# Order of a load queue: keys of the second tile against pieces of weights

## The reference, cut to what matters

```python
out_d = sm_attn(q_d, k_d, v_d)            # q, k, v averaged over 4 positions
out_up = np.repeat(out_d, factor, axis=2)
mask = np.abs(pos[:, None] - pos[None, :]) < factor
...
out_local = np.matmul(attn, v)
x = out_up + out_local                    # to (2304, 512)
xn = x / rms * rms_g
x = (silu(xn @ w_gate) * (xn @ w_val)) @ w_out          # 512 -> 1536 -> 512
r = np.maximum(x @ w_in, 0.0)
out = (s * (r * r) + b) @ w_out2                        # 512 -> 2048 -> 512
```

## Time and profile before

| | |
|---|---|
| runs | 1056.06, 1056.22, 1058.25 us; median 1056.22 |
| the profiled execution | 1057.01 us, of which 1054.9 us are the span of the trace |
| PE busy | 968.6 us (92%) |
| DVE, ACT, POOL busy | 529.8, 329.9 and 411.5 us |
| TensorE's granted clock, mean | 0.979 of full speed |

### The profile page before, as it was taken

One profiled execution on the slowest core, in us unless ns is written; L12 is line 12 of the kernel. 1 busy time (PEld: TensorE's weight loads), 2 busy tenths in 40 slices (PEclk: granted clock), 3 DMA queues, 4 the chain that ended last, 5 costly groups with the idle time before them and its releaser, 6 DMA issues.

```text
span 1054.9 us, 12788 instructions
## 1 busy us (share of the span) xinstructions
PE 968.6 (92%) x4864; PEld 772.0 (73%) x4864; DVE 529.8 (50%) x785; ACT 329.9 (31%) x706; POOL 411.5 (39%) x216
## 2 busy tenths in 40 slices
PE   5398977694999999999999999999999999999997
PEld 4276666583667767777777889787888888888896
DVE  4578774485667567556553222334343443343343
ACT  3233652223332243233323244423222232222222
POOL 4887974486578658747460055300000000000000
PEclk9999988897999999999999999999999999999999
DMA  9986423341142213301100343201100200010010
GB/s 262 284 227 185 131 77 122 93 143 39 46 142 61 61 53 102 92 18 39 58 25 1 120 141 120 80 1 40 41 1 1 80 1 1 21 40 0 1 41 20
DMA packets 54376, 79.38 MB, mean 75 GB/s; under 512 B 9836, under 2 KB 37068, under 8 KB 52908
## 3 DMA queue, kind: packets, MB, share of 16 engines
q1 hardware_dynamic: 53212, 73.86, 23.8%
q10 hardware_dynamic: 1104, 4.72, 1.1%
HBM read 67.05 MB, written 11.50 MB: 74 GB/s over the span
## 4 chain that ended last, share of the span: by engine, by line
PE 75%; POOL 8%; DVE 6%; DMA 4%; issue 3%; ACT 2%; SPq 2%; ACTq 0%; DVEq 0%; POOLq 0%
PE bank L726 22%; PE bank L848 6%; PE bank L866 6%; PE bank L850 6%; PE bank L849 6%; PE bank L867 6%; PE bank L868 6%; PE bank L762 4%; PE bank L760 4%; POOL prod L531 4%; PE bank L761 4%; DMA ks<-in_k_dram 2%; POOL prod L545 2%; DMA rawk<-in_k_dram 2%; PE bank L1477 1%
## 5 line engine op out<-in xcount | busy, mean ns | idle before, releaser
L531 POOL TENSOR_TENSOR prod<-qs,ks 128x896 f32<-128x896 f32 x80 | 174.8, 2209 | 106.7 <-DVE sc L551 63.0
L545 POOL TENSOR_TENSOR prod<-sc,vs 128x896 f32<-128x896 f32 x80 | 151.3, 1988 | 60.8 <-DVE x L561 43.4
L887 DVE SCALAR_TENSOR_TENSOR r<-bank,r 128x512 f32<-128x512 f32 (+1 forms) x80 | 51.1, 638 | 183.8 <-ACT r L875 183.8
L850 PE MATMUL bank<-y_h,w2i_l 128*128 128x512 f32 (+1 forms) x320 | 117.9, 368 | 0.0
L551 DVE TENSOR_REDUCE sc<-prod 128x14 f32<-128x896 f32 x80 | 85.5, 1079 | 59.4 <-POOL prod L531 59.4
L726 PE MATMUL bank<-x_h,wg_h 128*128 128x512 f32 (+1 forms) x264 | 90.5, 363 | 22.5 <-ACT u L770 22.3
L726 PE MATMUL bank<-x_h,wv_h 128*128 128x512 f32 (+1 forms) x264 | 102.2, 398 | 9.0 <-DVE h_l L788 9.0
L782 DVE TENSOR_TENSOR bank<-bank,u 128x512 f32<-128x512 f32 (+1 forms) x66 | 39.5, 599 | 132.2 <-PE bank L726 123.3
L760 PE MATMUL bank<-h_h,wo_h 128*128 128x512 f32 (+1 forms) x264 | 104.3, 395 | 0.0
L875 ACT ACTIVATE r<-bank 128x512 f32<-128x512 f32 (+1 forms) x80 | 44.4, 555 | 183.8 <-PE bank L850 183.0
L561 DVE TENSOR_REDUCE x<-prod 128x128 f32<-128x896 f32 x80 | 85.8, 1079 | 18.9 <-POOL prod L545 18.6
(11 more groups left out here) (131 smaller groups left out, 1924.6 us busy)
## 6 DMA issues: line engine op xcount, KB each, us to landing
raww<-in_moe_w_out_dram SPq DMA_DIRECT2D x14, 512.0 KB, 3.7
ks<-in_k_dram SPq DMA_DIRECT2D x16, 280.0 KB
vs<-in_v_dram SPq DMA_DIRECT2D x16, 280.0 KB, 5.1
y_scr<-y_st ACTq DMA_DIRECT2D x4, 1024.0 KB, 3.9
raww<-in_moe_w_in_dram SPq DMA_DIRECT2D x8, 512.0 KB, 4.1
y_raw<-y_scr SPq DMA_DIRECT2D x4, 1024.0 KB, 4.8
out_dram<-o_st SPq DMA_DIRECT2D x16, 256.0 KB, 2.8
rawq<-in_q_dram SPq DMA_DIRECT2D x3, 1152.0 KB, 10.6
```

The lines of the kernel that those rows point to most:

```text
L531: pool.tensor_tensor(dst, qv, kv, ALU.mult).then_inc(prod_ready, 1)
L545: pool.tensor_tensor(dst, pv, vv, ALU.mult).then_inc(prod_ready, 1)
L850: last = pe.matmul(o, w2i_l[:, m, kk, :], y_h[t % 2][:, kk, 0:w], start=False, stop=kk == DT - 1)
```

## The change

The order of the loads in SyncE's queue is changed between the load of head 2 of tile 1 and piece 14. The transfers, their waits and the lists of all other engines are the same.

```diff
             load_qk(sp, 1, 2)
+            load_qk(sp, 1, 3)
             load_piece(sp, 7)
-            load_qk(sp, 1, 3)
             load_qk(sp, 1, 4)
+            load_qk(sp, 1, 5)
             load_piece(sp, 8)
+            load_piece(sp, 9)
             store_co(3)
-            load_piece(sp, 9)
-            load_qk(sp, 1, 5)
+            load_qk(sp, 1, 6)
             load_piece(sp, 10)
+            load_qk(sp, 1, 7)
             load_piece(sp, 11)
-            load_qk(sp, 1, 6)
+            load_qk(sp, 2, 0)
             load_piece(sp, 12)
-            load_qk(sp, 1, 7)
+            load_qk(sp, 2, 1)
             load_piece(sp, 13)
-            load_qk(sp, 2, 0)
-            load_qk(sp, 2, 1)
             load_piece(sp, 14)
```

## The result

The changed kernel takes 1033.45 us (median of 4 runs, 1031.43 to 1034.91) against 1056.33 us for the kernel before (4 runs, 1056.06 to 1058.25): ratio 0.978, 95% interval 0.976 to 0.980. Repeated beside later experiments, it gave 1030.8 against 1054.9 us and 1032.31 against 1057.46 us, ratios 0.977 (0.976 to 0.978) and 0.976 (0.974 to 0.978). The three differences are 22.9, 24.1 and 25.2 us; 25.1 was forecast, 1031 us as the time.

The account below looks back on a forecast made before the run. POOL's 31.6 us of waits for keys, loaded late by queue order, bound the stage before TensorE's busy stretch. Plain gain 27.4 us, 25.1 net of POOL-DVE blocking: 1056.2 - 25.1 = 1031.1, called 1031 us; range 1024 to 1039.

Parts of the forecast that it names:

- The circle: Tile 1's key loads: load, product, reduce, low part, piece, next load delay each other; POOL waits 31.6 us for keys.
- Its links: Forecast times along the loads of heads 3, 5, 6, 7 and tile 2's head 0, taking 5.7 us per load.
- What comes back: POOL and DVE block each other in tile 1, at product 14 and line 582, cutting the gain from 27.4 to 25.1 us.
- plain sum of 27.4 us: Gain at tile 1's last reduce before POOL-DVE blocking: 31.6 of waits less 0.6, 2.3, 0.7 and 0.6 us.
- The first rival: POOL never blocks DVE's line 582 or the reverse; gain 27.4 to 31.6 us, 1024.6 to 1028.8 us; chance 0.17.
- The 0.6 us: DVE's low part of piece 8 holds POOL's product 14 back from 170.3 to 170.9 us.
- its clock: TensorE's gaps mostly under 3 us, so no half-clock cost taken; other end one half-clock stretch, 1.5 to 3 us.
- second rival: Late head 7 load, half-clock TensorE or another collision replaces 4 to 8 us of waits; 1035 to 1039 us; chance 0.22.
- sign of being wrong: DVE waiting for TensorE's val in steps 4 to 9, head 7 landing in 8 us or more, or TensorE's start near 260 unmoved.
- The cover: Moved weight pieces stay hidden: pieces 8 and 9 ahead of need by over 8 us; piece 11 uncovered would cost 5.3.
- Reaching the end: After its 11.27 us gap ending at 260.66, TensorE starts 25 us earlier and its 98% busy stretch moves whole.

Follow-up runs that it names:

- the three partial orders: Old order with only head 3's load moved, or heads 3 and 5; changed order with head 6's load behind piece 11: 1053.36, 1047.35, 1040.55 us.
- e7_after_again: The changed kernel run again unaltered, as control on the chip of later experiments: 1030.8 us, ratio to the kernel before 0.9768.
- e9_after_third: The changed kernel run a third time unaltered, as control for POOL waiting for the whole softmax: 1032.31 us, ratio to the kernel before 0.9758.
- e4_pieces_late: Against the changed kernel, loads of heads 6 and 7 also put ahead of pieces 8 and 9: 1040.39 us, ratio to the kernel before 0.9844.
- e6_head7_first: Against the changed kernel, head 7's load put ahead of piece 10 too: 1031.52 us, ratio to the kernel before 0.9776.
- e3_head6_back: Against the changed kernel, head 6's load put back behind piece 11, head 7 and tile 2's head 0 behind it: 1040.55 us.
- e8_wait_probs: Against the changed kernel, POOL's first product of tile 2 waits for tile 1's whole softmax: 1034.79 us, ratio to the kernel before 0.9781.
- e5: Against the changed kernel, POOL's first product of tile 2 waits for line 582 of tile 1's softmax: 1031.19 us, ratio to before 0.9782.

## Why the prediction was right

Times from here on are counted as the prediction does, that is, those of the profile after less 2.97 us; rows and windows stand in their profile's own times.

- **The circle.** It named POOL's waits for keys (31.6 us) as the loss and the pieces ahead of the loads as their cause. They fell to 0.4, and the three partial orders (3.5, 9.6 and 16.4 us) show that each load put back brings its own delay. The sums made beforehand were 3.5, 9.5 and 18 to 20 us.
- **Its links.** Product 6 at 145.1 (145.0 forecast), product 11 ending at about 163.2 (163.1), DVE's low part of piece 6 ending at 164.3 (164.15), head 6's queries out at 156.8 (156.6), product 13 at 167.7 (167.5), head 7's queries at 164.7 (164.6), line 582 beginning at 178.55 (178.05), the two reduces over at 185.2 (184.75).
- **What comes back.** Of the plain sum of 27.4 us it took off 0.6 and 1.65 for POOL and DVE blocking each other. Line 582 took 1.77 us instead of 0.39, which is 1.4 us and not 1.65, and the experiments with a wait on POOL move that cost from one line to the other and away. The first rival, no such collision, fails at line 582 in all three profiles of the changed order (1.76 or 1.77 us each time).
- **The 0.6 us was in part luck.** In the first profile DVE's low part of piece 8 did hold product 14 back, by 1.1 us (5.26 us for two products, against 4.15). In the two repeats it was over when the keys of head 7 came, 6.3 and 6.7 us after their first issue instead of 5.7, and nothing was blocked:

```profile
169.97 4.20 POOL L531 TENSOR_TENSOR prod<-qs,ks 128x896 f32<-128x896 f32 x2 [1.14 <-DMA ks<-in_k_dram]
```

```profile
174.82 4.20 POOL L531 TENSOR_TENSOR prod<-qs,ks 128x896 f32<-128x896 f32 x2 [1.56 <-DMA ks<-in_k_dram]
```

  Product 14 ran 36.2, 35.9 and 36.3 us after product 2 in the three, and 35.8 was forecast. The sum held either way, as a late landing took the place of the block.
- **TensorE.** I took nothing for its clock. In the first profile it ran part of step 3 at half clock (1.2 GHz) after a gap of 2.50 us (granted 0.72 on average from 163.5 to 168 us), and DVE waited 0.35 and 0.82 us for val at steps 4 and 5. That is a small part of the second rival, and one of the things that the prediction had named as a sign of being wrong. In the two repeats the same gap was 2.52 us, the clock stayed full and DVE did not wait for val there. The three rows are of changed, e7_after_again and e9_after_third:

```profile
163.50:168.00 4.50, 2.56 (x12) 0.72 0.04 14
```

```profile
159.52:164.02 4.50, 2.57 (x22) 1.00 0.10 36
```

```profile
163.94:168.44 4.50, 2.59 (x22) 1.00 0.04 15
```

- **The missing 0.7 us** (24.4 in the stage against 25.1). 0.4 us are lost by the end of the two reduces and 0.3 behind them, where DVE's low part of piece 10 takes 2.64 us in all three profiles instead of 2.23. What the half clock cost is not shown: e9_after_third, at full clock, is 0.1 us longer in the stage than the first profile, e7_after_again 0.4 us shorter.
- **The cover.** Pieces 8 and 9 were said to stay ahead of need by over 8 us. That counts from the issue: in e4_pieces_late piece 8 went out 12.2 us later than in the changed kernel, counted from product 2, and ScalarE waited 7.6 us, so the cover was about 4.6 us.
- **Reaching the end.** From the end of its last gap on TensorE is as busy as before, so the stage's gain passed to the end whole.
- **The size on record** was off by 2.2 us in the first comparison (22.9 of 25.1) and by 1.0 and 0.1 in the next two. The three profiles of this one order begin product 2 at 138.10, 134.12 and 138.54 us: the landing of the first loads alone spreads an execution by 4 us. Their stages agree within 0.6 us. That the medians came so near 1031 is therefore partly luck; the stage is the surer check.

## What to carry to other kernels

In a queue that issues in order, look for the transfer whose own wait was met long before it went out, and ask whose wait stood ahead of it; where the late data feeds the engine that frees the slot of that other transfer, the delay is paid once in every round. Put each load where its wait is met, and check the ones it now holds up: two more loads ahead of two pieces gave back 6 to 8 us. Subtract what comes back once the engines run at the same time, and compare stages from a common event, since the start of an execution can spread more than the change in question.

## What the runs showed of the hardware

- GpSimd's and VectorE's tensor-by-tensor instructions, both with two float32 inputs in SBUF, did not run side by side: a DVE instruction of 0.39 us took 1.77 us under a product, one of 1.22 us took up to 2.95, and a product of 2.07 took about 3.2. A small difference in the start decided which one waited: DVE's low part of piece 8 held product 14 back where it began 0.1 us before it (e6_head7_first), and waited for it where it began 0.2 us behind it (e3_head6_back). This is the rule of the Trainium skill (SBUF — State Buffer, "Who interferes with whom"); the trace agrees.
- Not expected: the same first loads were there 3 us apart in two executions (27.47 and 30.41 us), and up to 4.8 us apart over all profiles (26.1 in e8_wait_probs, 30.9 in e9_after_third), which is more than the gap between several of the kernels compared here.
- The same gap of TensorE, 2.50 to 2.53 us, was followed by half clock in two profiles (granted 0.72 and 0.70 over 4.5 us, changed and e8_wait_probs) and by full clock in four (1.00, e5, e6, e7 and e9). What decides is not shown.
